# A hand-written order for VectorE in the first three weight chunks, with two casts moved

## The chip, the cores and the metric

The kernel runs on one core of one Trainium2 chip. The metric is the device time of one execution in microseconds (us), the median over several runs. The kernel before takes 904.4 us (three runs, 903.55 to 904.43). The execution that the profiler recorded took 903.96 us; its span, from the first to the last recorded instruction, is 901.3 us.

## The reference

Sliding-window attention feeds two MLPs. All tensors are float32; the attention has 4 batches, 8 heads, 576 positions and head size 64, so the MLPs see 2304 tokens of width 512.

```python
scores = scale * q @ k.T                       # masked to 0 <= i - j < 64
attn   = softmax(scores);  x = (attn @ v).reshape(2304, 512)
rms = sqrt(mean(x * x) + 1e-6);  xn = x / rms * rms_g
g = xn @ w_gate                                # 512 -> 1536
y = (g * sigmoid(g) * (xn @ w_val)) @ w_out    # 1536 -> 512
h = y @ w_in                                   # 512 -> 2048
return (h * sigmoid(1.702 * h)) @ w2_out       # 2048 -> 512
```

## The kernel before

**Stages.** The tokens of the first MLP go in five tiles t (256, then four of 512). The hidden width 1536 is cut into 12 chunks c of 128. For each chunk TensorE (PE) makes the gate product (`gate`), the value product (`val`), and, two chunks later, adds the chunk's output product (`project_A`). Every product is three float32r matmuls, of a high and a low part of both operands (lines 647 to 649). The second MLP follows and is not touched here.

**Attention in between.** Attention goes in steps s, each for two heads and 256 tokens. Steps 0 to 3 come ahead of the MLP. Steps 4 to 11 belong to tile 1 and are woven into tile 0, in pairs. For the pair (4, 5): PE makes the scores after `val(1)`; VectorE (DVE) takes the row maxima (`row_max`, eight blocks a pair, L1130); ScalarE (ACT) the exponentials (`exponentials`, L881); DVE the reciprocals and the multiplication (`reciprocal_of_sum`, `normalise`, L1140 to L1147). PE transposes the probabilities in chunk 3, behind `val(3)` (L614); ACT copies them out (`copy_probT`, L908); PE multiplies by V behind `project_A(1)` (`probs_by_v`, L628) and makes the scores of steps 6 and 7 behind that (L600). ACT copies the result out in chunk 4 (`evacuate_o`, L874), for which `val(4)` waits.

**Weights.** In tile 0 each chunk's three matrices m (0 gate, 1 value, 2 output; 256 KB each) come by DMA from SyncE (SP) into a staging buffer for two chunks (`load_wA`, L405). ACT casts m = 0 and 1 to the high part (`weights_hi_by_act`, L920), GpSimd (POOL) casts m = 2 (`weights_hi_A`, L546), and DVE subtracts to get the low part (`weights_lo_A`, L1215), which raises the semaphore `w_split`. The load of chunk c + 2 overwrites chunk c, so it waits until `w_split` has reached the place of (c, m) in the written order `FIRST_SPLITS`:

```python
if c >= 2:
    sp.wait_ge(w_split, splitsA(c - 2, m))
```

SP issues its DMAs in order: after the chunk 2 loads come chunks 3, 4 and 5, then q and k of steps 6 and 7, then chunk 6, chunk 7, and so on.

**Order of the work.** Nothing is planned by a program: each engine has its own instruction list, written out in the order in which the calls stand, and waits at semaphores. A waiting instruction holds everything behind it on its engine. ACT's list in tile 0 is: tanh 0 and 1 (L996), `hid_hi_A(0)` (L1006), casts of chunk 3; `hid_hi_A(1)`, casts of chunk 4; exponentials 4, tanh 2, exponentials 5, `hid_hi_A(2)`, casts of chunk 5; then tanh 3, `copy_probT` 4 and 5, `hid_hi_A(3)`, casts of chunk 6; then `evacuate_o` 4 and 5, exponentials 6. DVE multiplies the gate by the inverse RMS (`scale_gate`, L1246), makes the SiLU (`silu_A`, L1251), multiplies by the value product (`hidden_A`, L1260) and takes the low part (`hid_lo_A`, L1266). `project_A(0)` waits for `hidden_A(1)`, since its accumulators lie where chunk 1's value product was.

Of the kernel before, what the change touches and what calls it, by code (L numbers as in the profile page):

```python
# [23 lines left out]
def fused_attention_mlps(nc, q_t, k_t, v_win, w_a, rms_g, w_b, out):  # L24
# [5 lines left out]
    CA = w_a.shape[0]  # L30
# [36 lines left out]
    with ExitStack() as ctx:  # L67
# [205 lines left out]
        def raw(u, m):  # L273
            return wstage[:, (3 * u + m) * DM:(3 * u + m + 1) * DM]

        FIRST_SPLITS = ((0, 0), (0, 1), (1, 0), (1, 1), (2, 0), (0, 2), (2, 1), (1, 2), (2, 2))

        def splitsA(c, m):
            return FIRST_SPLITS.index((c, m)) + 1 if c < 3 else 3 * c + m + 1

        CASTS_BY_ACT = ((0, 1), (1, 1), (2, 0), (2, 1)) + tuple((c, m) for c in range(3, CA) for m in range(2))
        CASTS_BY_POOL = ((0, 0), (1, 0), (0, 2), (1, 2)) + tuple((c, 2) for c in range(2, CA))
# [585 lines left out]
        def _(act):  # L868
# [146 lines left out]
            for t in range(NA):  # L1015
                for c in range(CA):
                    scored = pair_with_scores_at(t, c - 1)
                    transposed = pair_with_scores_at(t, c - 2)
                    multiplied = pair_with_scores_at(t, c - 3)
                    if multiplied is not None:  # L1020
                        evacuate_o(multiplied)
                        evacuate_o(multiplied + 1)
                    if scored is not None:
                        exponentials(scored)
                    if (t, c) != (0, 1):
                        tanh_A(t, c)
                    if (t, c) == (0, 0):
                        tanh_A(0, 1)
                    if c == SUMSQ_AT and t + 1 < NA:
                        sum_hi(t + 1)  # L1030
                    if scored is not None:
                        exponentials(scored + 1)
                    if transposed is not None:
                        copy_probT(transposed)
                        copy_probT(transposed + 1)
                    hid_hi_A(t, c)
                    if c == SUMSQ_AT and t + 1 < NA:
                        inverse_rms(t + 1)
                    if t == 0 and c + 3 < CA:
                        weights_hi_by_act(c + 3, 0)  # L1040
                        weights_hi_by_act(c + 3, 1)
                    if t == NA - 1 and 4 <= c < 4 + COMBOS:
                        xcB_hi_block(0, c - 4)
                    if t == NA - 1 and c in (7, 9):
                        w2in_hi((c - 7) // 2, range(IN_PIECES))
                    if t == NA - 1 and c == CA - 1:
                        w2out_hi(0, 0)
                        w2out_hi(0, 1)
                if t < NA - 1:
                    act.wait_ge(val_done, CA * (t + 1))  # L1050
                    split_x_hi(t + 1)
                    if t > 0:
                        wait(act, x2_stored, 16 * t)
                        evacuate_A(t)
# [60 lines left out]
        def _(dve):  # L1115
# [20 lines left out]
            def reciprocal_of_sum(s):  # L1136
                dve.wait_ge(exp_done, s + 1)
                wait(dve, probs_normed, s - EARLY + 1)
                by = rrec[:, s % EARLY, :]
                nc.vector.tensor_scalar(by, rsum[:, s % EARLY, :], 1.0e-9, None, ALU.add).then_inc(rec_order, 1)  # L1140
                dve.wait_ge(rec_order, 2 * s + 1)
                nc.vector.reciprocal(by, by).then_inc(rec_order, 1)
# [67 lines left out]
            def weights_lo_A(c, m):  # L1210
                if cast_by_act(c, m):
                    dve.wait_ge(w_hi_by_act, casts_so_far(True, c, m))
                else:
                    dve.wait_ge(w_hi_made, casts_so_far(False, c, m))
                nc.vector.tensor_tensor(slotA(c)[:, m, 1, :], raw(c % 2, m), slotA(c)[:, m, 0, :].bitcast(F32),  # L1215
                                        ALU.subtract).then_inc(w_split, 1)
# [26 lines left out]
            def scale_gate(c):  # L1243
                dve.wait_ge(gate_done, c + 1)
                dve.wait_ge(rinv_ready, 1)
                nc.vector.tensor_tensor(scaled_of(c), gate_of(0, c), rinv0[:, :], ALU.mult).then_inc(gate_scaled, 1)  # L1246

            def silu_A(t, c):
                n, w = CA * t + c, TILES_A[t][1]
                dve.wait_ge(sigA_ready, n + 1)  # L1250
                nc.vector.scalar_tensor_tensor(out=silu_of(t, c), in0=silu_of(t, c), scalar=1.0,  # L1251
                                               in1=scaled_of(c) if t == 0 else gate_of(t, c),
                                               op0=ALU.add, op1=ALU.mult).then_inc(siluA_done, 1)

            def hidden_A(t, c):
                n, w = CA * t + c, TILES_A[t][1]
                dve.wait_ge(siluA_done, n + 1)
                dve.wait_ge(val_done, n + 1)
                wait(dve, hidA_lo, n)
                nc.vector.tensor_tensor(hid[:, 0:w], val_of(t, c), silu_of(t, c),  # L1260
                                        ALU.mult).then_inc(hidA_made, 1)

            def hid_lo_A(t, c):
                n, w = CA * t + c, TILES_A[t][1]
                dve.wait_ge(hidA_hi, n + 1)
                nc.vector.tensor_tensor(h_lo[:, c % RING, 0:w], hid[:, 0:w],  # L1266
                                        h_hi[:, c % RING, 0:w].bitcast(F32), ALU.subtract).then_inc(hidA_lo, 1)

            def evacuate_A(t):
                n = TILES_A[t][1]  # L1270
                for j in range(DC) if t == 0 else (1, 3):
# [8 lines left out]
                    else:  # L1280
                        nc.vector.tensor_scalar(x2stage(t)[:, j, 0:n], acc_of(t, j), 0.5, None,
                                                ALU.mult).then_inc(accA_evacuated[1], 1)

            for t in range(NA):
                for c in range(CA):
                    scored = pair_with_scores_at(t, c - 1)
                    if scored is not None:
                        row_max(scored)
                        row_max(scored + 1)
                    split = c + 2 if t == 0 and c + 2 < CA else None  # L1290
                    if t == 0 and c != 1:
                        scale_gate(c)
                    if t == 0 and c == 0:
                        scale_gate(1)
                        weights_lo_A(2, 1)
                    if scored is not None:
                        reciprocal_of_sum(scored)
                        normalise(scored)
                    if split is not None and c > 0 and c != 2:
                        weights_lo_A(split, 0)  # L1300
                    silu_A(t, c)
                    hidden_A(t, c)
                    if t == 0 and c == CA - 2:
                        dve.wait_ge(ones_ready, 1)
                        nc.vector.tensor_copy(ones_r[:, :], ones[:, :])
                    if c == SUMSQ_AT and t + 1 < NA:
                        dve.wait_ge(ss_hi_made, t + 1)
                        nc.vector.tensor_tensor(ss_lo[:, :], ss[:, :], ss_hi[:, :].bitcast(F32),
                                                ALU.subtract).then_inc(ss_split, 1)
                    if scored is not None:  # L1310
                        reciprocal_of_sum(scored + 1)
                        normalise(scored + 1)
                    if split is not None and c == 2:
                        weights_lo_A(split, 0)
                    if split is not None and c > 0:
                        weights_lo_A(split, 1)
                    if t == 0 and c == 0:
                        weights_lo_A(1, 2)
                    hid_lo_A(t, c)
                    if split is not None:  # L1320
                        weights_lo_A(split, 2)
                    if t == NA - 1 and 4 <= c < 4 + COMBOS:
                        if sum_at(c - 4) is not None:
                            sum_x2(0, sum_at(c - 4))
                        xcB_lo_block(0, c - 4)
                    if t == NA - 1 and c in (6, 8):
                        combine_w2((c - 6) // 2)
                    if t == NA - 1 and c in (7, 9):
                        w2in_lo((c - 7) // 2, range(IN_PIECES))
                    if t == NA - 1 and c == CA - 1:  # L1330
                        w2out_lo(0, 0)
                        w2out_lo(0, 1)
                if t < NA - 1:
                    dve.wait_ge(val_done, CA * (t + 1))
                    for d in range(DC):
                        split_x_lo(t + 1, d)
                    wait(dve, x2_stored, 16 * t)
                    evacuate_A(t)
# [122 lines left out]
```

## Time and profile before

| what | number |
|---|---|
| median of three runs | 904.4 us |
| profiled execution | 903.96 us |
| its span | 901.3 us |
| PE busy | 889.2 us (99%) |
| DVE busy | 539.1 us (60%) |
| ACT busy | 400.2 us (44%) |
| PE waits from 20 to 60 us | 4.8 us |
| PE waits from 91 to 880 us | none listed |

Each row of the timeline gives the start in us from the span's beginning, the duration in us, the engine, the line, the operation with its output and input, a count (an entry with x2 or more holds several instructions that follow one another) and, in brackets, how long the engine had been idle and what released it. An engine starts its next instruction a little before the recorded end of the last one, about 0.08 us on DVE; the text calls the distance between two starts the step.

### The profile page before, as it was taken

To read this page: it belongs to the slowest core of one execution; us is meant where nothing else is said; L and a number is where in the kernel's file an instruction comes from. 1 tells how busy PE (TensorE), PEld (TensorE's weight loads), DVE (VectorE), ACT (ScalarE), POOL (GpSimd) and SP (SyncE) were. 2 spreads that over 40 slices of the span, in tenths; PEclk is the share of its full clock that TensorE was granted. 3 is DMA by queue.
4 is the path that set the end of the run, shared out by engine and by line. 5 is a ranking of instruction groups with operands and counts; after the bars stand their busy time and mean duration, and the time that the engine had idled before them with its cause. 6 is when DMAs were issued, how large, how long until landed. Compare 5 with 4: busy or idle time off the path is not lost.

```text
span 901.3 us, 14698 instructions
## 1 busy us (share of the span) xinstructions
PE 889.2 (99%) x5368; PEld 771.5 (86%) x5368; DVE 539.1 (60%) x1256; ACT 400.2 (44%) x944; POOL 81.0 (9%) x111
## 2 busy tenths in 40 slices
PE   8899999999999999999999999999999999999998
PEld 7799888888888888888888899999999999999997
DVE  6896633334333343333336578887788788867663
ACT  6666333343333433334123354545464554545442
POOL 5234001030010300112000000000000000000000
PEclk9999999999999999999999999999999999999999
DMA  7673111102111021100500222121432121241201
GB/s 243 217 218 94 51 51 51 50 24 74 51 50 52 24 74 50 51 25 1 186 1 24 94 95 70 63 78 47 164 117 94 48 77 65 69 143 48 70 24 70
DMA packets 41078, 69.75 MB, mean 77 GB/s; under 512 B 3632, under 2 KB 13872, under 8 KB 41008
## 3 DMA queue, kind: packets, MB, share of 16 engines
q1 hardware_dynamic: 39600, 67.12, 22.9%
q10 hardware_dynamic: 1408, 1.70, 0.5%
q8 instruction: 43, 0.70, 0.3%
q14 instruction: 27, 0.22, 0.1%
HBM read 59.38 MB, written 9.44 MB: 76 GB/s over the span
## 4 chain that ended last, share of the span: by engine, by line
PE 93%; DVE 3%; ACT 2%; issue 1%; POOL 0%; ACTq 0%; POOLq 0%
PE ps L647 16%; PE ps L648 15%; PE ps L649 15%; PE ps L839 7%; PE ps L840 7%; PE ps L838 7%; PE ps L781 7%; PE ps L777 7%; PE ps L779 6%; PE ps L628 2%; PE ps L600 2%; PE ps L614 1%; DVE w_all L1215 1%; ACT prob L881 1%; DVE sig L1251 0%
## 5 line engine op out<-in xcount | busy, mean ns | idle before, releaser
L647 PE MATMUL ps<-x_hi,w_all 128*128 128x512 f32 (+1 forms) x480 | 179.3, 373 | 0.0
L649 PE MATMUL ps<-x_lo,w_all 128*128 128x512 f32 (+1 forms) x480 | 176.7, 368 | 0.0
L648 PE MATMUL ps<-x_hi,w_all 128*128 128x512 f32 (+1 forms) x480 | 176.7, 368 | 0.0
L840 PE MATMUL ps<-w2out,hB 128*128 128x512 f32 x288 | 113.0, 392 | 0.0
L839 PE MATMUL ps<-w2out,hB 128*128 128x512 f32 x288 | 112.9, 392 | 0.0
L838 PE MATMUL ps<-w2out,hB 128*128 128x512 f32 x288 | 112.0, 389 | 0.0
L647 PEld LDWEIGHTS ps<-x_hi,w_all 128*128 128x128 f32 x480 | 90.4, 188 | 18.1 <-issue 3.0
L649 PEld LDWEIGHTS ps<-x_lo,w_all 128*128 128x128 f32 x480 | 90.4, 188 | 15.3
L648 PEld LDWEIGHTS ps<-x_hi,w_all 128*128 128x128 f32 x480 | 90.4, 188 | 14.4
L1251 DVE SCALAR_TENSOR_TENSOR sig<-sig,ps 128x512 f32<-128x512 f32 x48 | 32.9, 686 | 107.1 <-ACT sig L996 107.1
L647 PE MATMUL ps<-h_hi,w_all 128*128 128x512 f32 (+1 forms) x240 | 90.4, 377 | 1.9 <-DVE hid L1260 1.7
L648 PE MATMUL ps<-h_hi,w_all 128*128 128x512 f32 (+1 forms) x240 | 88.9, 370 | 0.0
L649 PE MATMUL ps<-h_lo,w_all 128*128 128x512 f32 (+1 forms) x240 | 88.9, 370 | 0.0
L1260 DVE TENSOR_TENSOR hid<-ps,sig 128x512 f32<-128x512 f32 (+1 forms) x59 | 37.9, 642 | 66.3 <-PE ps L649 52.7
L781 PE MATMUL ps<-xcB_even,w2in 128*128 128x384 f32 x224 | 75.2, 336 | 0.0
L777 PE MATMUL ps<-xcB_even,w2in 128*128 128x384 f32 x224 | 75.2, 336 | 0.0
L1006 ACT CAST h_hi<-hid 128x512 fp32r<-128x512 f32 (+1 forms) x60 | 34.8, 580 | 90.8 <-DVE hid L1260 90.8
L779 PE MATMUL ps<-xcB_even,w2in 128*128 128x384 f32 x224 | 75.1, 335 | 0.0
L996 ACT ACTIVATE sig<-ps 128x512 f32<-128x512 f32 x48 | 28.6, 597 | 103.6 <-PE ps L649 103.4
L840 PEld LDWEIGHTS ps<-w2out,hB 128*128 128x128 f32 x288 | 54.0, 188 | 11.4
L839 PEld LDWEIGHTS ps<-w2out,hB 128*128 128x128 f32 x288 | 54.0, 188 | 10.4
L838 PEld LDWEIGHTS ps<-w2out,hB 128*128 128x128 f32 x288 | 54.1, 188 | 10.2
(148 smaller groups left out, 1556.0 us busy)
## 6 DMA issues: line engine op xcount, KB each, us to landing
wstage<-in_w_b SPq DMA_DIRECT2D x48, 512.0 KB, 3.5
wstage<-in_w_a SPq DMA_DIRECT2D x36, 256.0 KB, 3.3
vwin<-in_v_win SPq DMA_DIRECT2D x32, 256.0 KB, 3.7
kwin<-in_k_t SPq DMA_DIRECT2D x32, 160.0 KB, 3.3
x2raw<-x_scratch SPq DMA_DIRECT2D x3, 1536.0 KB, 6.7
out_dram<-yB SPq DMA_DIRECT2D x18, 256.0 KB, 4.5
qtok<-in_q_t SPq DMA_DIRECT2D x34, 128.0 KB, 2.6
x_scratch<-wstage SPq DMA_DIRECT2D x3, 1024.0 KB, 4.2
```

Source lines behind the costliest of these rows:

```text
L647: pe.matmul(out_, w[:, 0, cols], xh, start=first, stop=False, **flags)
L648: pe.matmul(out_, w[:, 1, cols], xh, start=False, stop=False, **flags)
L649: return pe.matmul(out_, w[:, 0, cols], xl, start=False, stop=last, **flags)
L777: pe.matmul(out_, w2in[:, g % 2, 0, a_, cols], x[:, b_, 0, d, :], start=fresh and d == 0, stop=False, skip_group_check=True)
L779: pe.matmul(out_, w2in[:, g % 2, 1, a_, cols], x[:, b_, 0, d, :], start=False, stop=False, skip_group_check=True)
L781: ins = pe.matmul(out_, w2in[:, g % 2, 0, a_, cols], x[:, b_, 1, d, :], start=False, stop=last, skip_group_check=True)
L838: pe.matmul(y, h[:, rows], w[:, 0, chunk, :], start=(p == 0 and first), stop=False)
L839: pe.matmul(y, h[:, rows], w[:, 1, chunk, :], start=False, stop=False)
L840: ins = pe.matmul(y, hB_of(g, chunk, 1)[:, rows], w[:, 0, chunk, :], start=False, stop=last)
L1006: nc.scalar.copy(h_hi[:, c % RING, 0:TILES_A[t][1]], hid[:, 0:TILES_A[t][1]]).then_inc(hidA_hi, 1)
L1251: nc.vector.scalar_tensor_tensor(out=silu_of(t, c), in0=silu_of(t, c), scalar=1.0, in1=scaled_of(c) if t == 0 else gate_of(t, c), op0=ALU. ...
L1260: nc.vector.tensor_tensor(hid[:, 0:w], val_of(t, c), silu_of(t, c), ALU.mult).then_inc(hidA_made, 1)
```

## The change

DVE's list for chunks 0 to 2 of tile 0 is written out, and the loop starts at chunk 3. In the new list `silu_A(1)` and `hidden_A(1)` move ahead of three weight splits; the row maxima and both normalisations of steps 4 and 5 are done before `silu_A(2)`; and the splits (2, 2), (3, 2) and all three of chunk 4 stand behind `hidden_A(2)`. `FIRST_SPLITS`, which the loads wait by, follows the new order. ACT casts (4, 0) and (4, 1) after `hid_hi_A(2)` instead of after `hid_hi_A(1)`. Nothing is added or removed: the number of instructions is the same on every engine.

DVE's order before, from the same place, was: scale 0, scale 1, split (2,1), silu 0, hidden 0, split (1,2), low 0, splits (2,2) and (3,0), silu 1, hidden 1, split (3,1), low 1, split (3,2), maxima 4 and 5, scale 2, normalise 4, silu 2, hidden 2, normalise 5, splits (4,0) and (4,1), low 2, split (4,2), scale 3.

```diff
-        FIRST_SPLITS = ((0, 0), (0, 1), (1, 0), (1, 1), (2, 0), (0, 2), (2, 1), (1, 2), (2, 2))
+        FIRST_SPLITS = ((0, 0), (0, 1), (1, 0), (1, 1), (2, 0), (0, 2), (2, 1), (1, 2), (3, 0), (3, 1),
+                        (2, 2), (3, 2), (4, 0), (4, 1), (4, 2))
-            return FIRST_SPLITS.index((c, m)) + 1 if c < 3 else 3 * c + m + 1
+            return FIRST_SPLITS.index((c, m)) + 1 if c < 5 else 3 * c + m + 1
...
-                    if t == 0 and c + 3 < CA:
+                    if t == 0 and c == 2:
+                        weights_hi_by_act(4, 0)
+                        weights_hi_by_act(4, 1)
+                    if t == 0 and c != 1 and c + 3 < CA:
                         weights_hi_by_act(c + 3, 0)
                         weights_hi_by_act(c + 3, 1)
...
+            scale_gate(0)
+            scale_gate(1)
+            weights_lo_A(2, 1)
+            silu_A(0, 0)
+            hidden_A(0, 0)
+            silu_A(0, 1)
+            weights_lo_A(1, 2)
+            hid_lo_A(0, 0)
+            hidden_A(0, 1)
+            weights_lo_A(3, 0)
+            weights_lo_A(3, 1)
+            row_max(EARLY)
+            hid_lo_A(0, 1)
+            scale_gate(2)
+            row_max(EARLY + 1)
+            reciprocal_of_sum(EARLY)
+            normalise(EARLY)
+            reciprocal_of_sum(EARLY + 1)
+            normalise(EARLY + 1)
+            silu_A(0, 2)
+            hidden_A(0, 2)
+            weights_lo_A(2, 2)
+            weights_lo_A(3, 2)
+            hid_lo_A(0, 2)
+            for m in range(3):
+                weights_lo_A(4, m)
+
             for t in range(NA):
-                for c in range(CA):
+                for c in range(3 if t == 0 else 0, CA):
```

Here `EARLY` is 4. In the loop the special cases for chunks 0 to 2 go; for chunks 3 to 11 its order is as before.

## Rows read from the trace of the kernel before

**Rows 1.** Page, busy time and share of the span by engine.

```profile
PE 889.2 (99%) x5368; PEld 771.5 (86%) x5368; DVE 539.1 (60%) x1256; ACT 400.2 (44%) x944; POOL 81.0 (9%) x111
```

**Rows 2.** Waits of PE, 20 to 60 us: total us, times, longest.

```profile
PE ps L614 <- DVE prob L1147: 2.6, 2, 1.6
```

**Rows 3.** Timeline of PE: `project_A(0)`, end of `val(3)`, transposes 4 and 5, `probs_by_v`.

```profile
29.02 0.35 PE L647 MATMUL ps<-h_hi,w_all 128*128 128x256 f32 x1 [1.67 <-DVE hid L1260]
...
33.28 0.28 PE L649 MATMUL ps<-x_lo,w_all 128*128 128x256 f32 x1
34.55 0.65 PE L614 MATMUL ps<-ident,prob 128*128 128x128 f32 x4 [0.99 <-DVE prob L1147]
36.77 1.04 PE L614 MATMUL ps<-ident,prob 128*128 128x128 f32 x4 [1.57 <-DVE prob L1147]
...
40.30 1.15 PE L628 MATMUL ps<-probT,vwin 128*64 128x64 f32 x32
```

**Rows 4.** Busy time by window; PEclk is TensorE's granted clock, last DMA's share, GB/s.

```profile
38.00:39.00 1.00, 1.00 (x7) 1.00 (x6) 1.00 (x3) 0.00 (x0) 0.00 (x0) 0.50 0.39 90
...
41.00:42.00 1.00, 1.00 (x39) 0.93 (x39) 1.00 (x3) 1.00 (x4) 0.00 (x0) 1.00 0.89 307
```

**Rows 5.** Timeline of DVE, 25 to 39 us.

```profile
25.41 0.68 DVE L1215 TENSOR_TENSOR w_all<-wstage,w_all 128x512 fp32r<-128x512 f32 x1
26.01 0.83 DVE L1266 TENSOR_TENSOR h_lo<-hid,h_hi 128x256 fp32r<-128x256 f32 x1
...
28.45 0.42 DVE L1260 TENSOR_TENSOR hid<-ps,sq 128x256 f32<-128x256 f32 x1
...
30.74 0.28 DVE L1130 CUSTOM_DVE_ANT_0 prob<-ps,mask 128x128 f32<-128x128 f32 x1
...
32.43 0.41 DVE L1246 TENSOR_TENSOR sig<-ps,hid 128x256 f32<-128x256 f32 x1
33.38 0.17 DVE L1140 TENSOR_SCALAR rrec<-rsum 128x4 f32<-128x4 f32 x1 [0.54 <-ACT prob L881]
...
33.80 0.69 DVE L1147 TENSOR_TENSOR prob<-prob,rrec 128x512 f32<-128x512 f32 x1
...
37.84 0.42 DVE L1266 TENSOR_TENSOR h_lo<-hid,h_hi 128x256 fp32r<-128x256 f32 x1
...
38.77 0.42 DVE L1246 TENSOR_TENSOR sig<-ps,hid 128x256 f32<-128x256 f32 x1
```

**Rows 6.** Timeline of ACT: casts of chunks 3 and 4, exponentials 4, tanh 2, copies.

```profile
26.73 1.26 ACT L920 CAST w_all<-wstage 128x512 fp32r<-128x512 f32 x2 [0.79 <-DMA wstage<-in_w_a]
...
30.37 0.62 ACT L920 CAST w_all<-wstage 128x512 fp32r<-128x512 f32 x1 [0.28 <-DMA wstage<-in_w_a]
31.70 0.40 ACT L881 ACTIVATE prob<-prob,nmax 128x128 f32<-128x128 f32 x1 [0.71 <-DVE nmax L1130]
...
33.26 0.40 ACT L996 ACTIVATE sig<-sig 128x256 f32<-128x256 f32 x1
...
39.55 1.06 ACT L908 COPY probT<-ps 128x512 f32<-128x512 f32 x2
...
41.97 0.64 ACT L874 COPY xT<-ps 128x256 f32<-128x256 f32 x2
```

**Rows 7.** Timeline of POOL: casts of (3,2), (4,2) and (5,2).

```profile
28.80 1.15 POOL L546 CAST w_all<-wstage 128x512 fp32r<-128x512 f32 x1 [2.23 <-DMA wstage<-in_w_a]
31.38 0.62 POOL L546 CAST w_all<-wstage 128x512 fp32r<-128x512 f32 x1 [1.43 <-DMA wstage<-in_w_a]
33.94 1.03 POOL L546 CAST w_all<-wstage 128x512 fp32r<-128x512 f32 x1 [1.94 <-DMA wstage<-in_w_a]
```

**Rows 8.** Timeline of SP: issue of loads (3,2); (4,1) and (4,2); (5,2).

```profile
26.12 0.33 SPq L405 DMA_DIRECT2D wstage<-in_w_a  x1
...
26.97 0.91 SPq L405 DMA_DIRECT2D wstage<-in_w_a  x2
...
30.85 0.33 SPq L405 DMA_DIRECT2D wstage<-in_w_a  x1
```

More of the change, by code:

```diff
@@ L1290, in _ @@
                     split = c + 2 if t == 0 and c + 2 < CA else None
-                    if t == 0 and c != 1:
+                    if t == 0:
                         scale_gate(c)
-                    if t == 0 and c == 0:
-                        scale_gate(1)
-                        weights_lo_A(2, 1)
                     if scored is not None:
@@ L1298, in _ @@
                         normalise(scored)
-                    if split is not None and c > 0 and c != 2:
+                    if split is not None:
                         weights_lo_A(split, 0)
@@ L1312, in _ @@
                         normalise(scored + 1)
-                    if split is not None and c == 2:
-                        weights_lo_A(split, 0)
-                    if split is not None and c > 0:
+                    if split is not None:
                         weights_lo_A(split, 1)
-                    if t == 0 and c == 0:
-                        weights_lo_A(1, 2)
                     hid_lo_A(t, c)
```

## The prediction

> **What bounds the kernel now.** I read the page first: PE is busy 889.2 of 901.3 us [rows 1], and from 91 to 880 us no wait of PE is listed. So a change in the first chunks can only move the point at which PE runs on without a gap, and everything behind it shifts by the same amount. Then the waits of PE: in the touched stretch it waits 2.6 us, in two parts, for the normalised probabilities of steps 4 and 5 [rows 2]. The timeline gives the places, 34.55 and 36.77 us, and one more: 1.67 us at 29.02 for `hidden_A(1)` [rows 3]. Last the granted clock: behind those gaps it is 0.50, the 1.2 GHz level, and at 41 us it is 1.00 again [rows 4]. At 40.30 us PE starts `probs_by_v(4)` without an idle entry [rows 3]. That is the point where I compare old and new.
>
> **What the front of the new order brings.** Steps are a row's duration less 0.08 us, except where two starts are subtracted. Up to 25.41 us nothing differs. From there DVE does silu 1 (0.35, an estimate from `scale_gate` and `hid_lo_A`, 0.42 and 0.42 long [rows 5]), split (1,2) (25.41 to 26.01, so 0.60 [rows 5]) and low 0. One of these also gives way to POOL's cast at 25.4 us: low 0 took 0.83 us next to it where 0.42 is its length alone [rows 5], so 0.41 is added once. Hence 25.41 + 0.35 + 0.60 + 0.41 = 26.77, low 0 with its result 0.45 later, and hidden 1 from 27.22 to 27.64 us. Before it started at 28.45 and PE followed 0.15 us after its end [rows 3, 5]. So `project_A(0)` starts at 27.79 instead of 29.02: 1.23 us gained.
>
> Those 0.41 us come back with each POOL cast that meets DVE. The Trainium skill, page "SBUF — State Buffer", section "Who interferes with whom", calls the port pair that VectorE and GpSimd share an exclusive lock. By that rule the same lock falls on whichever instruction now stands there; the number of casts is unchanged, so it changes no sum here, and its weight is that the cost moves and does not go.
>
> Splits (3,0) and (3,1) run from 27.56 to 28.76 us; ACT's two casts for them, 1.26 us from 26.73, end at 27.99 [rows 6], in time. Maxima 4: 28.76 to 29.61 (30.74 to 32.43 is 0.845 each [rows 5]). Exponentials 4 start 0.96 after the maxima start (31.70 less 30.74) and take 1.56 to the tanh [rows 5, 6]: 29.72 to 31.28. DVE meanwhile: low 1 with the POOL cast of (3,2) (0.34 + 0.41), scale 2 (0.34), maxima 5 (0.85), to 31.55. Reciprocal 0.42, normalise 4 ends 0.69 later, at 32.66, and the transposes of step 4 can start at 32.72 instead of 34.55. Exponentials 5 start at 31.66, behind tanh 2 and maxima 5, and end at about 33.30; reciprocal 5, normalise 5, end 34.45; transposes of step 5 at 34.51 instead of 36.77 [rows 3]. At this point PE is 2.26 us ahead. It does the four transposes (0.45) and `project_A(1)`, 12 matmuls of 0.12 us (36 matmuls less one from 29.02 to 33.28 [rows 3]), and reaches `probs_by_v(4)` at 36.4 us if its clock has stayed up.
>
> **What the back of it costs.** `probs_by_v(4)` waits for ACT's copy, and that is no longer in time. Split (2,2) stood right behind low 0 and was done by 27.5 us (26.01 + 0.76 + 0.68); now it stands behind hidden 2. Normalise 5 releases DVE at 34.37, silu 2 and hidden 2 take 0.80, and split (2,2) ends at 35.85 us. The load of (4,2) waits for it, and SP works in order: the loads of (5,0) and (5,1) stand behind it, with splits that were long done. Two issues take SP 0.91 us [rows 8], so 0.46 to 0.47 apiece. So (4,2) goes out at 35.88, (5,0) at 36.35, (5,1) at 36.8 us; before, (5,2), the last of the three of chunk 5, went out at 30.85 [rows 8]. From issue to use a lone load takes 2.68 us (26.12 to 28.80) and (5,2) took 3.09 (30.85 to 33.94) [rows 7, 8]; loads behind one another land 1.0 us apart (30.37 and 31.38 [rows 6, 7]), or closer by the 307 GB/s of the window at 41 us, 0.85 us for 256 KB [rows 4]. I take 0.9: (4,2) at 38.56, (5,0) at 39.45, (5,1) at 40.35.
>
> ACT has, behind hid_hi 2 (35.3 us), casts (4,0) and (4,1), whose loads are long in, to 36.5, and then casts (5,0) and (5,1), ahead of tanh 3 and the two copies. It stands still from 36.5 until (5,0) lands. Cast (5,1) 40.35 to 40.87, tanh 3 to 41.18, the first copy 0.58, and PE starts `probs_by_v(4)` at 41.9 us: 1.6 later than 40.30. DVE also waits, at split (4,2), for POOL's cast of a load landing at 38.56, so 39.2; with scale 3 at 39.9 (38.77 before [rows 5]) it is not the later of the two. Bounds: a load time of 2.68 for (5,1) too, without queueing, gives 41.0, 0.7 late; landings 1.0 apart and 0.4 more for the first, 42.5, 2.2 late. Mine lies between because the three are issued back to back, as those at 30.37 and 31.38 were.
>
> Now the next wait: `val(4)` needs `evacuate_o` 4 and 5, and ACT does those behind casts (6,0) and (6,1). Their loads follow (5,2) and 576 KB of q and k on SP, issued at 39.6 and 40.1; landing at 0.9 us for 256 KB, (5,2) 41.25, q and k 43.3, (6,1) 45.1. Cast to 45.7, two copies (0.64 [rows 6]) to 46.4, `val(4)` at 46.5. Before, the two L628 and L600 groups took 2.12 us from 40.30 and the gate 1.43, so `val(4)` was at 43.85: 2.6 late. And the clock: PE idles from 36.4 to 41.9, over three times the longest gap before (1.67), after which the granted clock was at 0.50 in the window at 38 us and at 1.00 in that at 41 us [rows 4]: PE had gone on at 36.77, so the slow stretch lasted 2.2 to 4.2 us from there. I take 3.8. If as much at half clock follows 41.9, up to 1.9 us go; `val(4)` is then at 47.3, 3.5 late. Before, the slow stretch lay ahead of 40.30 and is in that number. The clock's cost and ACT's wait overlap, so the two are not added: +2.6 to +3.5, of which I take +3.0, halfway, since the small matmuls at 41.9 lose less than half. Low ends: +0.7 if neither the second wait nor the clock costs anything; high end: 2.2 + 1.9 + 0.8 (casts of chunk 6 later still) = +4.9.
>
> From there the loop is as before; maxima 6 wait for PE's scores in both, so DVE and ACT shift with PE, and none of the gap of 0.5 us at 52.73 is used up. The profiled execution would take 903.96 + 3.0 = 906.96 us, and the median of the runs lies 0.44 above the profiled one: 904.4 + 3.0 = 907.4 us.
>
> The Trainium skill, page "TensorE: Matmul & The Clock Gate", section "What's actually happening", has the array at half rate after it was idle until it has been busy again for a while. By that rule the 5.5 us of idleness would cost its half-rate stretch in full, with the value nearer 907.9; the rows agree that it fell after shorter gaps.
>
> **The rivals.**
> A, 907.4, chance 0.68: as above.
> B, 904.0, 0.11: the loads of chunk 5 are there in time (or something lets SP pass (4,2)), and PE is held by DVE instead. It decides at whether (5,1) lands before 38.6 us, which needs split (2,2) 1.7 us earlier or a load in 1.8 us. Against: no load in rows 7 and 8 took under 2.68. Then scale 3 stands behind two splits, low 2 and three splits, 3.3 us after 35.17, at 38.5, tanh and copy bring 39.9: 0.4 ahead.
> C, 902.1, 0.05: the 2.26 us at the transposes stay. It would need the copies at 36.4 us, while scale 3 cannot be before 38.5 by the count above; only a wrong reading of the order would give it.
> D, 909.0, 0.16: the stall spreads. Casts (6,0), (6,1), then (7,0), (7,1) wait too, the clock is low twice, +4.6. For it: SP's queue is behind until chunk 7. Against: from chunk 6 on the loads wait for splits of the same period, as before, and the lag is not handed on.
>
> **Numbers.** About 0.2% (1.8 us) is what a measurement of this kernel tells from no change. Slower by more: all of D and nine tenths of A plus a little, 0.79; within: B and A's low tail, 0.15; faster: C and a part of B, 0.06. A's own range is 905.8 to 908.8; with a part of D and the low bound I give 905.0 to 909.2.
>
> **What would show it.** Right: PE's wait at `project_A(0)` falls from 1.67 to about 0.4 and the transposes of step 5 start near 34.5; (4,2) is issued at 35.9; ACT waits over 2 us for a DMA before a cast at about 39.4; PE waits some 5 us for L908 and starts L628 near 41.9; the granted clock is 0.50 behind it. Wrong: the load of (4,2) leaves before 34 us, or PE's wait at L628 stays under 2 us.

## The result and the profile after

The changed kernel took 907.68 us against 904.17 us (six runs each); the ratio is 1.0039, 95% interval 1.0029 to 1.0050. In a second comparison it was 1.0043 (1.0031 to 1.0056). It is 3.5 to 4.1 us slower; the forecast was 907.4, 3.0 us slower. The profiled execution took 907.03 us with a span of 904.4, against 903.96 and 901.3.

The page of the profile gives the same instruction counts and nearly the same busy time of PE, so the added time is idle time.

```profile
span 904.4 us, 14698 instructions
...
PE 888.7 (98%) x5368; PEld 771.4 (85%) x5368; DVE 539.6 (60%) x1256; ACT 400.2 (44%) x944; POOL 79.3 (9%) x111
```

The waits of PE from 20 to 60 us after the change (total, times, longest), to be set beside [rows 2]: both waits that the new order aims at have shrunk, and the one for ACT's copies, 0.5 us before, has grown to 5.9 us.

```profile
PE ps L629 <- ACT probT L909: 5.9, 2, 5.2
PE ps L615 <- DVE prob L1151: 1.4, 2, 1.2
PE ps L648 <- DVE hid L1264: 0.5, 1, 0.5
```

Together they are 7.8 us, where they were 4.8: 3.0 of the 3.1 us by which the span has grown.

The timeline of PE after, at the places of [rows 3] (lines have moved by one on PE): `project_A(0)`, transposes of step 4 and 5, `probs_by_v` 4 and 5, scores 6 and 7, the first matmul of gate 4.

```profile
27.86 0.36 PE L648 MATMUL ps<-h_hi,w_all 128*128 128x256 f32 x1 [0.54 <-DVE hid L1264]
...
32.64 0.66 PE L615 MATMUL ps<-ident,prob 128*128 128x128 f32 x4 [0.23 <-DVE prob L1151]
34.48 0.66 PE L615 MATMUL ps<-ident,prob 128*128 128x128 f32 x4 [1.19 <-DVE prob L1151]
...
41.72 1.98 PE L629 MATMUL ps<-probT,vwin 128*64 128x64 f32 x32 [5.15 <-ACT probT L909]
43.63 1.90 PE L601 MATMUL ps<-kwin,qtok 64*64 64x128 f32 x32
45.45 0.39 PE L648 MATMUL ps<-x_hi,w_all 128*128 128x256 f32 x1
```

At 34.48 PE is 2.29 us ahead of [rows 3]; seven us later it is 1.42 behind. The reason is on ACT. Its timeline after: casts (4,0) and (4,1), then (5,0) and (5,1), both of which waited for a DMA, then tanh 3 and the two copies.

```profile
35.57 1.14 ACT L921 CAST w_all<-wstage 128x512 fp32r<-128x512 f32 x2
39.18 0.62 ACT L921 CAST w_all<-wstage 128x512 fp32r<-128x512 f32 x1 [2.47 <-DMA wstage<-in_w_a]
40.17 0.62 ACT L921 CAST w_all<-wstage 128x512 fp32r<-128x512 f32 x1 [0.37 <-DMA wstage<-in_w_a]
40.69 0.41 ACT L997 ACTIVATE sig<-sig 128x256 f32<-128x256 f32 x1
41.01 1.05 ACT L909 COPY probT<-ps 128x512 f32<-128x512 f32 x2
```

The load that these are queued behind is (4,2). The timeline of SP shows it leaving at 35.85 us (in [rows 8] it is the second of the two from 26.97), with two of the next right behind it in the entry from 36.22, and POOL's cast of it 2.70 us after the issue, having idled for 8.44:

```profile
35.85 0.33 SPq L406 DMA_DIRECT2D wstage<-in_w_a  x1
...
36.22 0.91 SPq L406 DMA_DIRECT2D wstage<-in_w_a  x2
```

```profile
38.55 0.61 POOL L547 CAST w_all<-wstage 128x512 fp32r<-128x512 f32 x1 [8.44 <-DMA wstage<-in_w_a]
```

Windows of the kernel after (busy of PE, PEld, DVE, ACT, POOL, then granted clock, DMA share, GB/s) show the clock at the 1.2 GHz level from within PE's idle time on to 45 us, where [rows 4] had it back at 1.00 by 41.

```profile
36.00:38.00 2.00, 0.57 (x5) 0.37 (x4) 1.96 (x4) 0.71 (x2) 0.00 (x0) 1.00 0.53 133
...
40.00:41.00 1.00, 0.00 (x0) 0.00 (x0) 0.82 (x2) 0.83 (x2) 0.06 (x1) 0.50 1.05 381
...
44.00:45.00 1.00, 1.00 (x28) 1.00 (x24) 0.00 (x0) 0.25 (x1) 0.00 (x0) 0.50 1.06 399
...
46.00:47.00 1.00, 1.00 (x11) 1.00 (x10) 1.00 (x11) 1.00 (x6) 0.68 (x2) 1.00 0.76 246
```

The kernel before has a slow stretch as well. It lies ahead of `probs_by_v(4)`, in `project_A(1)`. The first and the last of its twelve matmuls in the kernel before:

```profile
37.46 0.56 PE L647 MATMUL ps<-h_hi,w_all 128*128 128x256 f32 x1
...
39.96 0.41 PE L649 MATMUL ps<-h_lo,w_all 128*128 128x256 f32 x1
```

and in the changed kernel:

```profile
34.90 0.36 PE L648 MATMUL ps<-h_hi,w_all 128*128 128x256 f32 x1
...
36.29 0.28 PE L650 MATMUL ps<-h_lo,w_all 128*128 128x256 f32 x1
```

Between the two starts lie 2.50 us before and 1.39 after. The four transposes ahead took 0.69 us (36.77 to 37.46) and 0.42. So the slow clock cost 1.4 us ahead of `probs_by_v(4)` in the kernel before and 1.6 us behind it after (3.73 us from 41.72 to 45.45, against 2.12 from 40.30 to 42.42): it has moved, and what makes the two kernels differ is nearly all PE's idle time.

The scores of step 7 end at 45.53 us instead of 42.48, 3.05 later, and the span is 3.1 longer: in this execution nothing is handed back afterwards.

### The profile page after: what moved, and what is told of

Its sections match the earlier page's. It is cut to its first block, busy times and chain, and to the rows that moved or that the text cites. A ratio compares the mean times of both kernels' runs of the same rounds, so it can differ in the third digit from the quotient of the medians.

```text
span 904.4 us, 14698 instructions
## 1 busy us (share of the span) xinstructions
PE 888.7 (98%) x5368; PEld 771.4 (85%) x5368; DVE 539.6 (60%) x1256; ACT 400.2 (44%) x944; POOL 79.3 (9%) x111
## 4 chain that ended last, share of the span: by engine, by line
PE 93%; ACT 2%; DVE 2%; issue 1%; DMA 1%; POOL 1%; POOLq 0%; DVEq 0%; ACTq 0%; SPq 0%
PE ps L648 16%; PE ps L650 15%; PE ps L649 15%; PE ps L840 7%; PE ps L841 7%; PE ps L839 7%; PE ps L782 6%; PE ps L778 6%; PE ps L780 6%; PE ps L629 2%; PE ps L601 2%; PE ps L615 1%; DMA wstage<-in_w_a 1%; ACT prob L882 1%; DVE w_all L1219 1%
```

## The experiments

Line numbers differ by some lines between kernels. Each ratio is to the kernel before, measured beside it.

**One split moved back into a gap.** The only change to the changed kernel:

```diff
             normalise(EARLY)
+            weights_lo_A(2, 2)
             reciprocal_of_sum(EARLY + 1)
...
             hidden_A(0, 2)
-            weights_lo_A(2, 2)
```

> The changed kernel with one line moved: split (2,2) stands between normalise 4 and reciprocal 5, where VectorE waited 0.74 us for the exponentials (33.32 us in the changed kernel's trace), instead of behind hidden 2. Theory (the late load of (4,2) and what SP issues behind it hold ScalarE): (4,2) leaves near 33.1 instead of 35.85 us, cast (5,1) runs near 37.8, PE starts probs_by_v(4) at 39.5 to 40.0 us instead of 41.72, and most of the loss goes: 904.0 to 905.5 us. Rival (the new order is slow for another reason, the delayed casts of chunk 4 or the crowding of splits behind hidden 2): the time stays within 0.8 us of 907.7.

Measured: 905.07 us, ratio 1.0016 (1.0007 to 1.0025). PE's wait fell from 5.15 to 3.21 us and `probs_by_v(4)` started at 39.88, as the theory has it. One line gives back more than half of the loss (0.0023 of 0.0039 by the ratios), and the intervals of the two kernels do not meet.

**The same split moved late in the kernel before.**

```diff
-        FIRST_SPLITS = (..., (2, 1), (1, 2), (2, 2))
+        FIRST_SPLITS = (..., (2, 1), (1, 2), (3, 0), (3, 1), (3, 2), (2, 2))
...
+                    if t == 0 and c == 2:       # behind hidden_A(0, 2)
+                        weights_lo_A(2, 2)
...
-                    if split is not None:
+                    if split is not None and c > 0:
                         weights_lo_A(split, 2)
```

> The kernel before with one split moved: (2,2) stands behind hidden 2, as in the change, and the written order of the loads follows; all else, ScalarE's casts of chunk 4 too, is as before. Theory: this alone gives the loss. (4,2) leaves near 35.7 us, ScalarE waits for (5,0) until 39.0, probs_by_v(4) starts near 41.6, total +2.5 to +3.3 us over the kernel before, 906.7 to 907.5. Rival (the loss needs the rest of the new order): under +1 us.

Measured: 907.02 us, ratio 1.0037 (1.0024 to 1.0051), as much as the whole change. The timeline of SP in this kernel has (4,2) leaving at the same time as in the changed one:

```profile
35.89 0.33 SPq L406 DMA_DIRECT2D wstage<-in_w_a  x1
```

ACT cast (5,0) and (5,1) at 39.22 and 40.67, the second 0.5 us later than in the changed kernel, and PE started `probs_by_v(4)` at 42.22, later than the 41.6 expected. It had waited only 3.20 us for it, since without the new front it had got there later. So the late split is sufficient for the loss, without the new front and with ACT's casts of chunk 4 at their old place.

**The slow clock by itself.** Spare matmuls fill most of PE's wait:

```diff
+                    if t == 0 and c == 3:
+                        pe.wait_ge(gate_scaled, 3)
+                        keep_busy(4, 20)
                     if transposed is not None:
                         probs_by_v(transposed, CA * t + c)
```

> The changed kernel with 20 spare 128-column matmuls on PE, into the idle bank 4, ahead of probs_by_v(4), about 4.9 us of the 5.15 us that PE idles, so that the granted clock doesn't fall. Theory A (the slow clock is a cost of its own, 1.6 us in probs_by_v and the scores): the scores of step 7 end 1.6 us earlier and the total falls by 1.2 to 1.8 us, to about 906.2. Theory B (ScalarE, held by the loads of chunk 6 until 45.9 us and free for exponentials 6 at 46.57, is nearly as late, so the clock is hidden behind it): PE waits at val(4) instead and the total falls by 0 to 0.5 us.

Measured: 906.15 us, ratio 1.0027 (1.0017 to 1.0038). The time is as theory A has it, but the trace is not: ACT cast (5,0) at 40.34 us, and the scores of step 7 ended at 45.63, no earlier than in the changed kernel (45.53).

```profile
43.43 1.17 PE L629 MATMUL ps<-probT,vwin 128*64 128x64 f32 x32 [2.46 <-ACT probT L912]
```

> The changed kernel with the 20 spare matmuls ahead of probs_by_v(4), a second time: in its first profile the loads of chunk 5 had landed 1.2 to 1.7 us later than in the changed kernel's, so that trace didn't show what the clock is worth, while its median was 1.5 us lower. Theory A (the clock is a cost of its own): ratio to the kernel before 1.0025 to 1.003 again, the same 1.2 to 1.6 us under the changed kernel, and with landings as in the changed kernel the scores of step 7 end near 44 us. Theory B (ScalarE nearly as late): ratio 1.0036 or more.

Measured: 905.98 us, ratio 1.0023 (1.0015 to 1.0032). The clock was 1.00 in every window looked at from 26 to 54 us, and the two groups took 2.20 us instead of 3.81:

```profile
42.41 1.17 PE L629 MATMUL ps<-probT,vwin 128*64 128x64 f32 x32 [1.40 <-ACT probT L912]
43.51 1.10 PE L601 MATMUL ps<-kwin,qtok 64*64 64x128 f32 x32
```

Both runs lie 0.0012 to 0.0020 under the two ratios of the changed kernel, 1.1 to 1.8 us; they were not measured side by side with it, and the intervals overlap. Theory A fits both times, theory B fits neither. In this trace the scores ended at 44.61, later than the 44 expected: the cast of (5,0) began at 40.15 instead of 39.18. In both traces with spare matmuls this load came about 1 us later (40.34 and 40.15) than in the three without them and with the same late issue (39.18 and 39.11 in the changed kernel, 39.22 in the kernel before with the late split). Why stays open, so what the clock alone is worth is not cleanly separated. There was also little more to win: ACT's copies for `val(4)` ended at 46.02, and PE started `val(4)` at 46.11.

**The changed kernel again.**

> The changed kernel itself, unaltered, beside the others, so that each can be set against it on one chip. Both theories expect about 1.0035 to 1.004 times the kernel before, as measured first (1.0039).

Measured: 907.62 us, ratio 1.0043 (1.0031 to 1.0056). In its profile (907.92 us) cast (5,1) began at 40.95 instead of 40.17, though the cast of (5,0) was at 39.11, and `probs_by_v(4)` at 42.50. The 0.9 us between the two profiled executions can't be put down to this load alone, since the slow stretch lay elsewhere too. The clock was still at 1.00 from 40 to 41 us, fell just before PE went on, and stayed at 0.50 until 48 us, over the gate and the value product of chunk 4:

```profile
47.00:48.00 1.00, 1.00 (x7) 1.00 (x7) 1.00 (x11) 0.57 (x3) 0.77 (x3) 0.50 0.85 215
```

The transposes of step 6 came 4.9 us later than in the kernel before (54.58 against 49.71), the span only 3.9 us: here about 1 us was handed back, at the places where PE of the kernel before still waits (0.55 us at 52.73, for one).

**ACT's casts behind the copies.**

```diff
+                    if t == 0 and c == 3:          # behind copy_probT(5)
+                        weights_hi_by_act(5, 0)
+                        weights_hi_by_act(5, 1)
                     hid_hi_A(t, c)
...
-                    if t == 0 and c != 1 and c + 3 < CA:
+                    if t == 0 and c not in (1, 2) and c + 3 < CA:
```

> The changed kernel with ScalarE's casts (5,0) and (5,1) behind tanh 3 and both copies of the probabilities, so that they no longer hold these. Theory (two branches of one late load: without the casts, VectorE's split (4,2), which waits for the same load and ended its wait at 39.20, holds scale 3 at 39.81): tanh 3 at 40.2, probs_by_v(4) at 41.2 instead of 41.72, total lower by 0 to 0.6 us. Rival (ScalarE's queue order is what costs, the load alone is harmless): probs_by_v(4) before 40.3 and the total lower by 1.5 us or more.

Measured: 906.72 us, ratio 1.0033 (1.0021 to 1.0046), not clearly under the changed kernel. ACT idled all the same, now for DVE:

```profile
40.69 0.42 ACT L997 ACTIVATE sig<-sig 128x256 f32<-128x256 f32 x1 [3.54 <-DVE sig L1253]
```

`probs_by_v(4)` was at 41.72 again, in a trace in which `project_A(0)` had started 0.36 us later than in the changed kernel's (28.22 against 27.86). Set against that start it came 0.4 us earlier, where 0.5 was expected; it is a reading from one trace. The queue order on ACT is one of two branches of nearly equal length; the other goes through POOL's cast of (4,2) and DVE's split.

**SP's order alone.**

```diff
-                    if t == 0 and c + 3 < CA:
+                    if t == 0 and c == 1:
+                        load_wA(4, 0)
+                        load_wA(4, 1)
+                        load_step_qk(6)
+                        load_step_qk(7)
+                        load_wA(5, 0)
+                        load_wA(5, 1)
+                        load_wA(4, 2)
...
```

> The changed kernel with SP's order alone altered: the loads of q and k for steps 6 and 7, (5,0) and (5,1) are issued ahead of (4,2), since what they wait for is done long before; VectorE's and ScalarE's orders stay as in the change. Theory (most of the loss is that SP's blocked issue holds back loads whose own condition was met; the rest is VectorE's own wait at split (4,2)): ScalarE casts (5,0), (5,1) at 36.7 to 37.8 without waiting, split (4,2) still waits until 39.2, so probs_by_v(4) starts near 41.1 us, the loads of chunk 6 land 1.5 to 2 us earlier, total lower than the changed kernel by 0.5 to 1.3 us. Rival (SP's order is the whole of it): probs_by_v(4) at 39.9 or before and the total within 0.9 us of the kernel before.

Measured: 905.99 us, ratio 1.0028 (1.0019 to 1.0037), 1.0 to 1.4 us under the changed kernel, though the intervals overlap. ACT's four casts ran in one entry from 35.60 without a wait, and `probs_by_v(4)` was at 41.34. Much of that gain is behind this point: casts (6,0), (6,1) ran at 42.09 in one entry, where the changed kernel waited 2.02 us for their loads. The rival needed 39.9 and fails.

**Both repairs.** The edits of the first and of the previous experiment together.

> Both repairs together: split (2,2) between normalise 4 and reciprocal 5, and SP's order as in the run with SP's order alone. Theory: no engine waits for a load of chunk 4 or 5 any more; scale 3 on VectorE, near 38.0, sets probs_by_v(4) at 39.3 us; PE still idles 2.9 us before it and some slow clock follows: total within 1.0 us of the kernel before (ratio 0.999 to 1.001). Rival (the front of the new order keeps its 2.26 us once the loads are out of the way): ratio 0.9975 to 0.9985.

Measured: 903.84 us, ratio 1.0001 (0.9992 to 1.0010). One of the eleven executions took 4501 us; the ratio leaves it out.

> Both repairs together (split (2,2) in the gap, SP's order), a second time, for a trace of it: the first profile was of a disturbed run. Expected as before: casts (5,0), (5,1) without a wait, scale 3 near 38.0, probs_by_v(4) at 39.3 us, slow clock behind it, ratio 0.999 to 1.001.

Measured: 903.60 us, ratio 0.9994 (0.9986 to 1.0003). No cast waited, and PE waited 3.36 us at 39.86 for the copy, which scale 3 on DVE set. That is 0.6 us later than the 39.3 expected, and the slow clock expected behind it did not come. What is left of the new order, with both repairs, is no gain that can be measured, though PE was 2.35 us ahead at the transposes of step 5 (34.42).

**Scale 3 early.** On top of both repairs:

```diff
             hidden_A(0, 2)
+            scale_gate(3)
...
+                    if t == 0 and c == 2:          # ahead of hid_hi_A(2)
+                        weights_hi_by_act(4, 0)
+                        weights_hi_by_act(4, 1)
...
+                    if t == 0 and c == 3:          # behind copy_probT(5)
+                        weights_hi_by_act(5, 0)
+                        weights_hi_by_act(5, 1)
```

> The previous one, and scale 3 right behind hidden 2 on VectorE, ScalarE's casts (4,0), (4,1) ahead of hid_hi 2, and its casts (5,0), (5,1) behind the copies of the probabilities, so that these copies wait for nothing but the transposes. Theory (VectorE, busy nearly throughout chunks 2 to 9, bounds how far PE can run ahead): probs_by_v(4) starts near 36.7 us and the clock stays at 1.00, but PE gives the lead back in waits for VectorE in chunks 4 to 9, and the total is 0.3 to 1.3 us under the kernel before (ratio 0.9986 to 0.9997). Rival (PE is the bound of the whole tile): the full 3.6 us stay, ratio 0.996.

Measured: 903.06 us, ratio 0.9993 (0.9984 to 1.0002). `probs_by_v(4)` started at 36.65, 3.65 us ahead of [rows 3], and almost all of it was lost at `val(4)`, which waits for `evacuate_o`, on ACT behind `hid_hi_A(3)`, which had waited 2.54 us for DVE, and casts (6,0) and (6,1), which waited 0.66 us for their loads. The profile names no releaser:

```profile
43.54 0.36 PE L656 MATMUL ps<-x_hi,w_all 128*128 128x256 f32 x1 [3.06 <-issue]
```

The clock, expected to stay at 1.00, was at 0.50 behind this wait, from 45 to 48 us.

**Steps 6 and 7 early.** On top of that:

```diff
+                        evacuate_o(4)          # ACT, ahead of hid_hi_A(3)
+                        evacuate_o(5)
...
+                    if (t, c) == (0, 3):       # ACT, ahead of the casts of chunk 6
+                        exponentials(6)
...
+                    if (t, c) == (0, 3):       # DVE, ahead of split (5,1)
+                        row_max(6)
...
+                    if (t, c) == (0, 3):       # DVE, behind hid_lo_A(3)
+                        row_max(7)
```

> The version with scale 3 early, and in it the pair of steps 6 and 7 drawn ahead: evacuate_o 4 and 5 and exponentials 6 before ScalarE's casts of chunk 6, row maxima 6 and 7 before and behind low 3 on VectorE. In the version with scale 3 early PE waited 3.06 us at val(4), for evacuate_o, which stood behind casts (6,0), (6,1) and their loads, and VectorE waited 0.92 us for exponentials 6. Theory (VectorE's own work is the bound, so only its idle time can be won): PE's wait at val(4) goes but is given back in later waits; 0.5 to 1.5 us under the kernel before (ratio 0.9983 to 0.9995). Rival (those waits were PE's bound): ratio under 0.9975.

Measured: 903.18 us, ratio 0.9988 (0.9979 to 0.9997): 1.1 us under the kernel before, the one version that beats both, by little. The wait at `val(4)` is gone and another has come, for normalise 7 on DVE:

```profile
36.65 1.17 PE L637 MATMUL ps<-probT,vwin 128*64 128x64 f32 x32
...
46.09 0.60 PE L623 MATMUL ps<-ident,prob 128*128 128x128 f32 x4
48.82 0.66 PE L623 MATMUL ps<-ident,prob 128*128 128x128 f32 x4 [2.13 <-DVE prob L1166]
```

**The same without SP's order.** SP's list as in the changed kernel.

> The previous version with SP's order as in the changed kernel: q and k of steps 6 and 7, (5,0) and (5,1) again stand behind (4,2), which now leaves at 33.1 us. Theory (with scale 3, the copies and the evacuation ahead of the casts, a load that lands by 38 us holds nothing on PE's path but the scores of step 6, whose q and k are issued near 36.5 and land near 40): PE waits 1 to 2 us at the scores of step 6 (they could start at 37.8), and the total is 0.3 to 1.5 us above the previous version. Rival (the order of SP no longer matters once (4,2) leaves early): equal within 0.3 us.

Measured: 905.19 us, ratio 1.0014 (1.0005 to 1.0023), 2.3 us above the previous version by the ratios, more than expected. PE waited for k of step 6, issued only behind (4,2) and chunk 5:

```profile
41.27 1.64 PE L601 MATMUL ps<-kwin,qtok 64*64 64x128 f32 x32 [3.31 <-DMA kwin<-in_k_t]
```

The expectation had 1 to 2 us of wait; I had let k land near 40, and it landed above 41. The clock fell behind this wait too, which I had not counted.

## Why the prediction was right

**The front.** 27.79 us was said for `project_A(0)`, 27.86 measured; transposes of step 4 at 32.72 against 32.64; those of step 5 at 34.51 against 34.48. The gain of 2.26 us was there (2.29) and was lost. POOL's cast fell on the instruction that now stood there, as said: split (1,2) took 1.10 us in place of 0.68, and low 0 behind it 0.41 in place of 0.83.

```profile
25.72 1.10 DVE L1219 TENSOR_TENSOR w_all<-wstage,w_all 128x512 fp32r<-128x512 f32 x1
```

**The load.** (4,2) out at 35.88, measured 35.85; its cast at 38.56, measured 38.55. (5,0) and (5,1) at 39.45 and 40.35, measured 39.18 and 40.17. `probs_by_v(4)` at 41.9, measured 41.72. That this chain is the cause, and not only what ended last in one trace, is shown from both sides: putting the split into a gap takes off more than half, and moving it late in the kernel before gives all of the loss within the noise.

**Two branches.** The prediction put DVE's wait at split (4,2) second, with scale 3 at 39.9 (39.81 measured). The run with ACT's casts behind the copies shows the margin: freed of the first branch, PE gains 0.4 us in one trace.

**What was off: the terms between 41.9 and the gate of chunk 4.** I wrote that "the small matmuls at 41.9 lose less than half". They took 3.73 us from 41.72 to 45.45, against 2.12 before, so 1.61 us were lost. That is 43% of the stretch, and so less than half of it, but it is most of the 1.9 that I had as the upper end. For the second wait ACT's part was read well: the two copies were said to end at 46.4 and ended at 46.58. The wait came to nothing all the same, since the slow clock brought PE there only at 46.9. At the end of the scores the late start (1.42) and the slow clock (3.81 us less 2.18, so 1.63) make the 3.05 measured. I had taken 3.0 as the middle between 2.6, from a wait that did not occur, and 3.5, from a start 1.6 late and 1.9 for the clock. The path up to 41.9 was right; that the 3.0 behind it fits the trace so closely is partly luck. The medians differ by 3.5 and 4.1, toward the top of the likeliest case or beyond it. That "none of the gap of 0.5 us at 52.73 is used up" held in the first profile of the changed kernel, where PE waited 0.79 us at this place, and not in the second, where it did not wait.

**Rivals.** B's 904.0, with the loads in time and DVE's scale 3 as the holder, is what both repairs give: 903.84 and 903.60, at 39.86 instead of the 39.9 written. C, that the 2.26 us stay, was tried by bringing the copies forward to 36.65: the lead came and was given back in chunks 4 and 5, so that about 0.1% is left. D's second stall was seen in part (ACT waited 2.02 us for chunk 6), but it lay behind the slow clock.

**The rule on the clock.** PE idled 5.15 us, the granted clock was 0.50 from within that idle time until 45 to 46 us, and filling the gap with spare matmuls kept it at 1.00; these kernels were lower by 1.1 to 1.8 us. The Trainium skill, page "TensorE: Matmul & The Clock Gate", section "What's actually happening", has the array at half rate after idle time until PE has been busy for a while. Both traces of the changed kernel agree; the trace with both repairs, 3.36 us idle and no fall, shows that such a gap need not be enough. The value that I set beside it, 907.9, is 3.5 us over the kernel before, my own 3.0; measured were 3.5 and 4.1, so the rule's was the nearer.

## What to carry to other kernels

When an instruction moves later on one engine, look for what waits on its semaphore from a DMA queue, and then for all that stands behind that issue in the same queue, whose own conditions may long be met: here one 0.6 us subtraction moved 8 us later held back six further loads, two engines and then PE. An early gain on the bounding engine is kept only if the next hand-over (here ACT's copy behind scale 3) comes forward as well; and where the second engine has hardly any idle time in the stretch, expect little. DVE was busy 21.73 of the 24 us from 36 to 60 us in the kernel before, and the best version won 1.1 us. That DVE's own work is the bound there fits these numbers, but no run removed any of that work, so it is not shown.

## What the runs showed of the hardware

The same gap at the same place need not bring the clock down. In the run with the split in the gap, PE idled 3.21 us until 39.88 and then ran at 0.50; in that with both repairs it idled 3.36 us until 39.86 and stayed at 1.00. The window from 41 to 42 us, of the first and of the second:

```profile
41.00:42.00 1.00, 1.00 (x21) 0.88 (x22) 1.00 (x3) 0.06 (x1) 0.00 (x0) 0.50 0.85 283
```

```profile
41.00:42.00 1.00, 1.00 (x33) 0.83 (x33) 1.00 (x3) 1.00 (x3) 0.16 (x1) 1.00 0.83 238
```

The two kernels differ in SP's order besides, and there is one such trace of each. But the mean granted clock of the other executions shows that the order of the work does not decide it alone. Over the whole execution it is 0.998 for the profiled one of the kernel before, with its one slow stretch, and 1.00 for the profiled one with both repairs, where the clock never fell. It was 1.00 in 33 of 77 executions of the kernel before, in 4 of 21 with both repairs (the one of 4501 us left out), in none of 11 with the split in the gap, in none of the 11 of the changed kernel, and in 17 of 18 with spare matmuls (0.999 in the other). So the same kernel loses the clock in one execution and keeps it in the next; what decides it stays open.

Small matmuls feel the clock as much as larger ones: 64 matmuls (L629, L601) took 3.73 us, nearly all of it at 0.50, and 2.12 at 1.00, a factor of 1.76. The eleven steps between the twelve 256-column matmuls of `project_A(1)` took 2.50 us in the kernel before and 1.39 after, a factor of 1.80. And the time between two landings of equal 256 KB loads issued back to back was 0.99 us in one profile of the changed kernel and 1.84 in another (casts at 39.18 and 40.17; at 39.11 and 40.95); in the kernel before with the late split it was 1.45 (39.22 and 40.67).
